# Keys and queries of the second sequence as 32 x 32 squares turned by VectorE, and one DMA per tile's norm

## What is computed

```python
batch, n_heads, seq, head_dim = (2, 8, 768, 64); n_sink, window = (4, 128)
scores = scale * q @ k.T ; keep = is_sink | in_window
a = softmax(where(keep, scores, -1e9)) ; x = (a @ v) as [1536, 512]
for e in range(4):   # experts, w1 [4, 512, 1024], w2 [4, 1024, 512]
    out += p[:, e] * (relu(x @ w1[e]) @ w2[e])
h = out @ w_in ; result = (h * cos(h)) @ w_out     # 512 -> 2048 -> 512
```

## Time and profile before

| | us |
|---|---|
| median of three runs | 833.78 (833.62 to 834.0) |
| the profiled execution, its own time | 837.64 |
| its span | 835.9 |
| TensorE busy | 831.0 |
| VectorE, ScalarE, GpSimd busy | 455.7, 458.0, 551.7 |

### The profile page before, as it was taken

The page is one execution under the profiler, slowest core; times in us unless marked ns, Lnnn a source line. Parts: engine busy times, 40 slices in busy tenths (PEclk is TensorE's granted clock), DMA queues, the critical chain, the costliest instruction groups (busy, mean ns, idle before and its releaser), DMA issues.

```text
span 835.9 us, 13778 instructions
## 1 busy us (share of the span) xinstructions
PE 831.0 (99%) x4564; PEld 743.6 (89%) x4564; DVE 455.7 (55%) x947; ACT 458.0 (55%) x985; POOL 551.7 (66%) x417
## 2 busy tenths in 40 slices
PE   9999999999999999999999999999999999999998
PEld 7777989988988988988988998998998998998997
DVE  4988833523523427633433433338767749756756
ACT  5888734334334435433423523525867869867864
POOL 3777996476476778575475575878384399685450
PEclk9999999999999999999999999999999999999999
DMA  8785231211221220432331131130223430530202
GB/s 184 169 190 147 67 123 51 102 61 44 98 68 44 91 83 19 117 105 53 95 112 50 52 101 51 51 101 30 73 63 76 125 117 0 177 102 18 84 1 76
DMA packets 101045, 70.46 MB, mean 84 GB/s; under 512 B 68368, under 2 KB 74864, under 8 KB 100976
## 3 DMA queue, kind: packets, MB, share of 16 engines
q1 hardware_dynamic: 100976, 69.58, 28.5%
HBM read 62.96 MB, written 3.19 MB: 79 GB/s over the span
## 4 chain that ended last, share of the span: by engine, by line
PE 96%; DVE 1%; issue 1%; ACT 1%; DMA 0%; SPq 0%; ACTq 0%; DVEq 0%
PE scores L1499 11%; PE scores L1503 11%; PE scores L1501 11%; PE scores L1512 10%; PE scores L1514 10%; PE scores L1510 10%; PE bank L1512 5%; PE bank L1514 5%; PE bank L1510 5%; PE bank L1499 3%; PE bank L1501 3%; PE bank L1503 3%; PE scores L1406 2%; PE bank L1441 2%; PE bank L1417 1%
## 5 line engine op out<-in xcount | busy, mean ns | idle before, releaser
L665 POOL TENSOR_TENSOR w_lo<-w_raw,w_hi 128x512 fp32r<-128x512 f32 x96 | 129.8, 1362 | 139.0 <-ACT w_hi L814 139.0
L1499 PE MATMUL scores<-x_hi,w_hi 128*128 128x384 f32 x528 | 177.1, 335 | 0.4 <-DVE x_lo L1136 0.2
L1503 PE MATMUL scores<-x_hi,w_lo 128*128 128x384 f32 x528 | 176.8, 335 | 0.0
L1501 PE MATMUL scores<-x_lo,w_hi 128*128 128x384 f32 x528 | 176.5, 334 | 0.0
L672 POOL TENSOR_TENSOR w_lo<-w_raw,w_hi 128x1024 fp32r<-128x1024 f32 x48 | 116.2, 2431 | 65.4 <-ACT w_hi L824 65.4
L824 ACT ACTIVATE w_hi<-w_raw 128x1024 fp32r<-128x1024 f32 x48 | 50.9, 1060 | 190.2 <-PE scores L1514 188.8
L1514 PE MATMUL scores<-w_hi,h_lo 128*128 128x512 f32 x384 | 149.3, 389 | 0.0
L1512 PE MATMUL scores<-w_lo,h_hi 128*128 128x512 f32 x384 | 149.3, 389 | 0.0
L1510 PE MATMUL scores<-w_hi,h_hi 128*128 128x512 f32 x384 | 149.0, 388 | 0.0
L1240 DVE SCALAR_TENSOR_TENSOR acc<-scores,probs,acc 128x512 f32<-128x512 f32 x56 | 41.8, 749 | 116.5 <-PE scores L1514 116.5
L1499 PEld LDWEIGHTS scores<-x_hi,w_hi 128*128 128x128 f32 x528 | 99.1, 188 | 2.4 <-issue 0.7
(11 more groups left out here) (140 smaller groups left out, 1548.0 us busy)
## 6 DMA issues: line engine op xcount, KB each, us to landing
w_raw<-in_moe_w_dram SPq DMA_DIRECT2D x30, 1024.0 KB, 5.1
w_raw<-in_moe_w_in_dram SPq DMA_DIRECT2D x8, 1024.0 KB, 5.0
w_raw<-in_moe_w_out_dram SPq DMA_DIRECT2D x8, 1024.0 KB, 5.4
v_nat<-in_v_dram SPq DMA_DIRECT2D x12, 256.0 KB, 4.0
norm<-routing_dram SPq DMA_DIRECT2D x24, 128.0 KB, 3.2
x_t<-t_sum SPq DMA_DIRECT2D x192, 16.0 KB, 1.9
k_nat<-in_k_dram SPq DMA_DIRECT2D x11, 256.0 KB, 3.8
q_nat<-in_q_dram SPq DMA_DIRECT2D x11, 256.0 KB, 3.6
```

Of the source, the lines that this page charges most:

```text
L665: nc.gpsimd.tensor_tensor(w1_slots(w1_lo, h % 2, part), w1_part(h % 2, part), w1_slots(w1_hi, h % 2, part).bitcast(F32), ALU.subtract)\
L1499: nc.tensor.matmul(target[:, 0:HALF], w1_hi[:, i, slot, d], x_hi[:, n - 1, d], start=first and d == 0, stop=False, skip_group_check=True)
L1501: nc.tensor.matmul(target[:, 0:HALF], w1_hi[:, i, slot, d], x_lo[:, n - 1, d], start=False, stop=False, skip_group_check=True)
L1503: last = nc.tensor.matmul(target[:, 0:HALF], w1_lo[:, i, slot, d], x_hi[:, n - 1, d], start=False, stop=d == 1, skip_group_check=True)
```

## The change

1. The keys and queries of the second sequence (tiles 6 to 11) are no longer loaded tile by tile and no longer turned by TensorE. Sixteen DMAs, eight for keys and eight for queries, bring all of them as rows of 32 floats (128 bytes): each DMA writes 32 partitions of 48 x 32 floats, 1,536 packets, 192 KB. Keys go into `x_t[:, 1]`, queries into a new tile over memory that `x_lo` uses later. Then one VectorE transpose of 32 x 32 squares per tile (`copy_keys`, and `turn_queries` for all six tiles) puts them where the scores read them. With these loads a pair of heads is h and h+2, not h and h+1; `head_at` and `sum_at` keep account of it.
2. The row sums are stored in that order, so that a tile's norm is read back with one DMA: 128 partitions of one row of 2,048 bytes each, from a source that is 2 rows, each read 64 times.
3. The first two sums of tokens, `sum_tokens(0)` and `(1)`, move from VectorE (rounds 18 and 20) to GpSimd (rounds 17 and 19). The last two stay on VectorE.

```diff
+            def load_squares(first, last):
+                for n in range(first, last):
+                    which, n = divmod(n, SQUARE_PARTS)
+                    dst, src = ((k_squares, k), (q_squares, q))[which]
+                    half, r, f = n // 4, n // 2 % 2, n % 2
+                    rows = slice((2 * r + f) * 32, (2 * r + f + 1) * 32)
+                    h = half * H // 2 + 2 * r
+                    source = src[1, h:h + 2, :, f * 32:(f + 1) * 32].rearrange("h s i -> (h s) i")
+                    target = dst[rows, 2 * half:2 * half + 2].rearrange("j p s -> j (p s)")
+                    sp.dma_start(target.rearrange("j (c i) -> j c i", i=32),
+                                 source.rearrange("(c j) i -> j c i", j=32))\
+                        .then_inc((k_squares_landed, q_squares_landed)[which], 16)
...
-                for r in range(2):
-                    sp.dma_start(norm[r * D:(r + 1) * D, t % 2],
-                                 sums_in_memory(t)[:, r].unsqueeze(0).broadcast_to([D, PAIRS, P]))\
-                        .then_inc(norm_landed[t % 2], 16)
+                sums = sums_in_memory(t).rearrange("(r p) s -> r (p s)", r=2)
+                sp.dma_start(norm[:, t % 2].rearrange("p k s -> p (k s)"),
+                             sums.unsqueeze(1).broadcast_to([2, D, PAIRS * P])).then_inc(norm_landed[t % 2], 16)
...
                 if t >= 3:
                     load_norm(t - 3)
-                if 5 <= t + 3 < T:
+                if 5 <= t + 3 < SQUARED:
                     load_keys(t + 3)
+                if t == 3:
+                    load_squares(6, 9)
+                elif t == 4:
+                    load_squares(11, 13)
                 if t >= 2:
                     store_inverse(t - 2)
-                if 5 <= t + 3 < T:
+                if 5 <= t + 3 < SQUARED:
                     load_queries(t + 3)
                 if 3 <= t < T:
                     load_values(t)
+                if t == 1:
+                    load_squares(0, 4)
+                elif t == 2:
+                    load_squares(4, 6)
+                elif t == 3:
+                    load_squares(9, 11)
+                elif t == 4:
+                    load_squares(13, 16)
...
+            def turn_queries(t):
+                dve.wait_ge(q_squares_landed, 16 * SQUARE_PARTS)
+                dve.wait_ge(scores_done, PAIRS * (t - 1))
+                n = t - SQUARED
+                nc.vector.transpose(q_t[:, t % 2], q_squares[:, :, n * P:(n + 1) * P]).then_inc(q_squares_ready, 1)
```

More of the change, by code:

```diff
@@ L51, in program @@
     ROUNDS = ND + VALUE_LAG
+    SQUARED = TPB
+    SQUARE_PARTS = 8
     KC = DM // P
@@ L110, in program @@
         x_hi = sb("x_hi", [P, 7, 2, HALF], F32R)
+        early = ExitStack()
+        sb("early_lo", [P, 2, 2, HALF], stack=early)
+        q_squares = sb("q_squares", [P, PAIRS, S], stack=early)
+        early.close()
         x_lo = sb("x_lo", [P, 7, 2, HALF], F32R)
@@ L186, in program @@
         first_landed = [sem("first_keys_landed"), sem("first_queries_landed")]
+        k_squares_landed = sem("k_squares_landed")
+        q_squares_landed = sem("q_squares_landed")
         probs_landed = sem("probs_landed")
@@ L204, in program @@
         q_ready = sem("q_ready")
+        q_squares_ready = sem("q_squares_ready")
         k_sink_kept = sem("k_sink_kept")
@@ L291, in prev_at, with head_at, sum_at @@
             return SLOT - own_at(t)
+        def head_at(t, n):
+            if t < SQUARED:
+                return n
+            half, at = divmod(n, H // 2)
+            p, r = divmod(at, 2)
+            return half * H // 2 + 2 * r + p
+        def sum_at(h):
+            return h % 2 * PAIRS + h // 2
         def heads(src, t):
@@ L300, in sums_in_memory @@
             at = t % TPB * rows
-            return routing[at:at + rows, :].rearrange("(p r s) e -> p r (s e)", p=PAIRS, r=2)
+            return routing[at:at + rows, :].rearrange("(h s) e -> h (s e)", h=H)
         def weights_of(s):
@@ L733, in _ @@
                     first_lo(1, i - ND)
+                if i in (17, 19):
+                    sum_tokens(0, (17, 19).index(i))
                 if i % 2 == 0 and 0 <= (i - 6) // 2 < T - 4:
@@ L923, in _ @@
                     exp_head(i, 3)
-                if i >= 2 and i % 2 == 0 and i // 2 + 1 < T and i // 2 + 1 not in QUERIES_BY_DVE:
+                if i >= 2 and i % 2 == 0 and i // 2 + 1 < SQUARED:
                     copy_queries(i // 2 + 1)
@@ L1048, in mask_head @@
                 n = 2 * j + r
[L1049 removed]
+                t, h = n // H, head_at(n // H, n % H)
                 if later(t):
@@ L1063, in copy_keys @@
             def copy_keys(t):
-                dve.wait_ge(k_turned, t + 1)
+                if t < SQUARED:
+                    dve.wait_ge(k_turned, t + 1)
+                else:
+                    dve.wait_ge(k_squares_landed, 16 * SQUARE_PARTS)
                 if t >= 3:
@@ L1152, in _ @@
                     copy_keys((i + 3) // 2)
-                elif i % 2 == 0 and i // 2 + 1 in QUERIES_BY_DVE:
-                    copy_queries(i // 2 + 1)
+                elif i % 2 == 0 and SQUARED <= i // 2 + 1 < T:
+                    turn_queries(i // 2 + 1)
                 if i % 2 == 0 and 0 <= (i - 2) // 2 < T:
@@ L1165, in _ @@
                     sum_weights(i - 7)
-                if i in (18, 20, 21, 23):
-                    sum_tokens((18, 20, 21, 23).index(i))
+                if i == 21:
+                    sum_tokens(2)
+                elif i == 23:
+                    sum_tokens(3)
                 if i == 22:
@@ L1390, in scores @@
                 else:
-                    pe.wait_ge(q_ready, t)
+                    if t < SQUARED:
+                        pe.wait_ge(q_ready, t)
+                    else:
+                        pe.wait_ge(q_squares_ready, t - SQUARED + 1)
                     pe.wait_ge(k_ready, t)
@@ L1582, in _ @@
                     turn_weights(i - TURN_LAG)
-                if i % 2 == 1 and (i + 3) // 2 < T:
+                if i % 2 == 1 and (i + 3) // 2 < SQUARED:
                     turn_keys((i + 3) // 2)
-                elif i >= 2 and i % 2 == 0 and i // 2 + 1 < T:
+                elif i >= 2 and i % 2 == 0 and i // 2 + 1 < SQUARED:
                     turn_queries(i // 2 + 1)
```

28 lines of the change are left out of this document (13 added, 15 removed).

## The result

The changed kernel takes 861.25 us (median of 6 runs, 858.02 to 864.59), the kernel before 833.97 (833.62 to 834.87): slower by a factor of 1.033, 95% interval 1.0303 to 1.0358. Forecast were 863.0 us, and a range of 836 to 878. The profiled execution took 864.28, its span is 862.6 us, 26.7 more than before.

The account below looks back on a forecast made before the run. TensorE, busy 831.0 of 835.9 us, was taken to bound the kernel. Late norms were to lengthen attention by 29.2 us, with the 5.2 us of transposes not gained: 833.8 + 29.2 = 863.0 us, range 836 to 878.

Parts of the forecast that it names:

- The norm on two engines: Norm DMA in attention: an outermost count of 2 puts it on two engines, 5.6 us, 8.5 a tile; chance 0.78.
- The rows without a landing: Profile page: only the two DMAs with outermost count 8 have no landing time, taken as sign that few engines carry them.
- The walk through the queue: DMA queue from 25.0 us: squares 1.3, loads 1.0, norms 5.6 us in order; norm 2 lands at 67.0, norm 7 at 109.5.
- rival 1: Attention: norm spread over 16 engines, squares late; 9 us lost, 5.2 won, 837.6 us; chance 0.11.
- Who waits: GpSimd in attention: norm 7 holds `normalise(7)`, then `part_weights(20)`, so `weigh_values(20)` starts at 112.0 instead of 82.77, 29.2 us longer.
- The token sums: GpSimd in attention: two sums at about 1.9 us bring it to 32.4 us, hidden as long as it isn't held up.
- The turns: TensorE in attention: twelve groups of four transposes leave, 0.435 us each, 5.2 us, not gained within the delay.
- rival 2: Attention: the change works, with norm on 16 engines and cheap squares; 829.6 us, up to 832 if VectorE bounds; chance 0.11.
- VectorE's wait for queries: VectorE's first transpose of queries: reached at 41.7, queries land at 61.5, a wait near 20 us.
- Rival 3: Norm chain in attention: two engines but squares cost little, period 7.6 us, +9, 843 us; chance 0.06, inside the 0.78.

Follow-up runs that it names:

- spread: The changed kernel with each norm as two DMAs of 64 rows instead of one, all else as changed: 846.23 us, 1.013 against the kernel before.
- split8: The kernel before with each load of keys and queries from tile 5 on issued as eight DMAs, same bytes and packets: 868.26 us, 1.039.
- norm_only: The kernel before with only the changed norm (one DMA), order of sums and store, no squares: 853.64 us, 1.021 against the kernel before.
- late_queries: On spread: queries of tiles 6 to 8 loaded in four DMAs and turned by TensorE, the other queries' squares issued later: 844.33 us, 1.010.
- half_two_queues: The kernel before with tiles 9 to 11 as squares in 32 DMAs of 384 packets, eight issued by ScalarE: 839.96 us, 1.007.
- wide_norm: norm_only with the norm as two DMAs of 64 rows, same bytes and order of sums, no squares: 836.05 us, 1.001 against the kernel before.

## Why the prediction was right

**The norm on two engines.** Right, and the main part. The rows without a landing pointed to it. Forecast were 5.6 us of packets and a gap of 2.9 until the next issue, 8.5 in all; measured are 7.9 us in the mean, of which issue to landing takes 7.2 to 8.5 (7.7 to 7.9 for the last three) and the gap 0.1. The two terms were wrong, and that their sum came near is luck: the 1.9 us that any DMA needs belong inside the norm's landing (7.8 less 1.9 over 64 packets is 92 ns, between my 84 and 100), and the store lands with the norm, not a DMA's time after it.

**The walk through the queue.** Norm 2 was to land at 67.0 and did at 65.50; the queries at 61.5, and VectorE's first transpose began at 60.40; norm 7 at 109.5, and it was 104.86. `weigh_values(20)` was to come 29.2 us late, it came 27.0 late. The walk gave each square 1.3 us of the DMA engines and counted nothing for SP, which was over its sixteen issues for 27.4 us (1.7 each); in this kernel the two fill each other, and the landings of the walk hold.

What the sum hid shows in rival 1: *norm over 16 engines, squares late* was priced at 837.6, and the kernel that does just that, spread, takes 846.2. Its landing was right too: the last square was to land at 51.7, and VectorE's first transpose of queries begins at 50.61. What follows it was wrong, 9 us to be lost and 5.2 won. Round by round against before, with the 3.4 us that spread is ahead at round 6 (22.14 for 25.59), TensorE is 11.4 us late at round 12 (53.93 for 45.94), 13.5 at round 17, and 12.1 at round 23. From 50 to 60 us its granted clock is 0.60. **The term that was mis-sized is the cost of lateness: norms come late as well as squares (GpSimd waits 16.7 us for norms in spread), and there is TensorE's lower level behind each wait, which the prediction put at nothing.** SP's time to issue was at nothing too. That this was wrong in principle is shown by split8; how much of the squares' cost in the change it makes, no run shows. SP's issues of one tile, added up from 28 to 57 us in the trace of before, already take 3.1 to 4.4 us of 6.4.

**Who waits.** This step failed, though the time came out near. I had norm 7 and `part_weights(20)` gate `weigh_values(20)`. The rows show the gate one norm earlier: norm 6 lands at 97.07, then come `normalise`, `part_weights`, the new token sum of 1.81 us and `gather_sinks` on GpSimd, and TensorE's `turn_sinks` waits for that until 102.09. From there it needs 7.7 us to `weigh_values(20)`, in part at the lower level. Norm 7's weights were parted at 107.3, 2.5 us before they were needed. That the other chain would have given nearly the same time is luck. The token sums, costed at nothing because GpSimd had room, lay on the path: once the norms were late, that cover was gone. All the gates are `turn_sinks` in odd rounds, five waits of 13.1 us together behind GpSimd, and one of 6.9 behind VectorE.

**The turns.** 5.2 us were to be won and lost within the waits. So it was. In spread most of the last four came out, 1.45 of 1.74 us; where the token sums stay on VectorE they don't, since VectorE becomes the bound. The prediction had that as "no slack left", and in rival 2 as up to 832 us.

**VectorE's wait for queries.** Forecast near 20 us, measured 9.1; VectorE was itself held until 51 by what TensorE lacked. The landing was right, the wait was not: a wait shows only the part that nothing else hides.

**The clock.** Not in the prediction at all. The four longer waits of TensorE in the kernel after (5.7, 6.9, 4.1 and 1.7 us) are each followed by 3 to 7 us of work at the lower level, wholly or in part. The matmuls at 46.27 and 48.17 alone cost 0.88 + 0.97 us more than at the higher. It is inside the 27.0 us; that the sum still fits is owed for the most part to the period, which the norms set whatever TensorE's clock.

**Rival 3** (the norm's chain alone, 843) was too cheap: norm_only, with no squares at all, takes 853.6, as its period is 8.8 and not 7.6 us. Norm alone +18 us, squares alone (spread) +11, both +27: the waits overlap a little, and each part alone makes the kernel slower.

## What to carry to other kernels

Before two DMAs are put into one, look at the outermost count of both sides: a broadcast that starts with 2 took some 7.9 us for 256 KB, with about two of 16 engines' worth of work in the DMA view, where two DMAs with 64 took 3.2 us each. Count what a queue's issuing engine needs for every DMA of a loop (here 0.3 to 0.6 us, and more where the queue held it) and hold it against the loop's period: with nothing else changed, more DMAs for the same bytes cost 33 us here while the DMA engines stood half idle. And before work leaves the bounding engine, see who is next: VectorE at 32.55 of 38 us was near enough to take the gain back wherever two token sums stayed on it.

## What the hardware showed that I had not expected

Where nothing held it, SP's issue of a DMA took 0.3 to 0.6 us, for a store of 4 KB as for a load of 256 KB in 1,024 packets. For 1,536 packets of 128 bytes it was 1.19 us in the median in the kernel after, 1.00 in spread and 0.81 in late_queries, 0.50 to 0.58 at least. For 384 packets SP took 0.47 us in the median in half_two_queues and ScalarE 0.32; the least of both is 0.32.

VectorE's token sums of 128x768 took 0.91 or 1.25 us in one and the same kernel. The rows of before show what each ran beside. The two of 0.91 us (67.16, 73.94) had begun before a GpSimd selection of weights, which then took 1.27 us for 0.63. The two of 1.25 us (77.80, 84.44) began while such a selection was running, and the next one took 1.35. So the two engines seem to keep each other out there, and a sum on VectorE costs GpSimd time too.

The granted clock fell during TensorE's waits and came back after 3 to 7 us of work, each matmul of that time taking up to twice as long. In wide_norm, where TensorE has no such wait, it stayed at 1.00, although the matmuls of its first 14 us took the times of the lower level, as before.
